# Routing tables in PSUM, a divisor out of the matmul, and another order of scatters and weight splits, in a fused attention and mixture-of-experts kernel

## The chip, the cores and the metric

The kernel runs on one core of a Trainium2 chip. The metric is the device time of one execution in microseconds.

## The reference

Three parts follow one another. Attention has 4 batches, 8 heads, 576 tokens, 64 columns; k and v are averaged over groups of 8 tokens first, so there are 72 keys.

```python
scores = scale * np.matmul(q, k_p.transpose(0, 1, 3, 2))
scores = scores - np.max(scores, axis=-1, keepdims=True)
attn = np.exp(scores)
attn = attn / (np.sum(attn, axis=-1, keepdims=True) + 1e-09)
return np.matmul(attn, v_p).astype(np.float32)
```

Its output is a matrix x of 2304 tokens by 512. Each token then goes to two of 8 experts: logits are `x @ w_gate`, plus noise times `log1p(exp(x @ w_noise))`; the two largest win; their weights are a softmax over the two. An expert is `relu(x @ w1) @ w2` with 1024 hidden columns. The last part is dense, with 2048 hidden columns: `h = x @ w_in`, then `max(0.01 * h, h) @ w_out`.

## The kernel before, in words

Every matmul of the experts and of the dense part is made of three (`halves3`, L663 to L667): each fp32 operand is split into a high half that TensorE takes exactly and the rest. Weights are split by GpSimd, in 16 chunks of 128x512 for each of ten stages (eight experts, two dense halves), out of a ring of four raw chunks (`w_raw`) that SP loads. A split is a TENSOR_SCALAR and a TENSOR_TENSOR (`split_chunk` L451, `split_next` L493). Activations are split by ScalarE and VectorE.

**Attention** works on 18 tiles of 128 tokens in a pipeline of steps: at step t TensorE scores tile t (`score`), turns the probabilities of t-1 and attends for t-2 (`attend`); VectorE centres t (`centre`: maximum and subtraction), pools k and v by reductions (`pool_k`, `pool_v`, L1026 and L1034) and normalises t-2 (`normalise`, L1050); ScalarE takes the exponentials and copies. The gate matrices are folded into the pooled v (`map_v`), so that `attend` gives each head's output, its share of the gate logits, and a column that sums the probabilities, since the last columns of `v_pool` hold 1.0. `normalise` adds 1e-9 to that sum and multiplies by 8 (L1053), takes the reciprocal (L1056), and makes the rows of x (L1058) and the products for the gates (L1062).

**Routing** goes by turns of 6, 5, 4 and 3 tiles, in four steps on VectorE: `gate` adds the products over the heads; `pick_first` (L1084) and `pick_second` (L1104) find the two experts, in 17 small operations, each waiting for the one before it (`link`); after TensorE's `rank` counts the picks, `place` (L1124) gives each row its slot in the DRAM buffer `x_sorted`, where every expert has a region. GpSimd then scatters the rows with one indirect DMA for each tile and pick (`send_rows`, L462), 36 in all, two at a time, with a weight split between pairs. The steps at which each part of a turn runs are in the tables at the end (L1384 to L1395); in a step of VectorE's loop (L1157) the order is centring, placing, pooling, normalising, gating, picking. The last turn's picks and placing come after the loop. Stage 1's split weights lie over `x_rows` in SBUF, so a chunk may be split only when the tile under it is sent.

**The order of the first blocks** is set by semaphores. SP waits until the scatters of turns 0 and 1 have landed, tells `early_landed`, loads two weight chunks, does the same for turn 2 (`mid_landed`), loads two more, and waits for turn 3 (L407 to L419). ScalarE loads the rows of block 0 and 1 after `early_landed`, block 2 after `mid_landed`, and all others after the last scatter (L933 to L958). VectorE works out the lists of blocks (L1215 to L1245) behind `split_rows(0)`, in one queue ahead of `split_h(0)`, on one partition of 45 x 8 elements for the larger ones. `need_rows` finds out whether a block's rows have been placed.

**Experts** follow as 43 blocks of 128 rows: `up`, the turning of the next rows (L672), `down` of the block before, `turn_h`. Their results go to `y_blocks`, and are gathered back and mixed during the dense part, which runs in five groups of tokens.

## Time and profile before

| | us |
|---|---|
| median of 3 runs | 1077.89 (1076.13 to 1080.1) |
| the profiled execution | 1074.86 |
| its span | 1072.8 |
| TensorE busy | 1035.0 |
| GpSimd busy | 380.1 |
| VectorE busy | 378.0 |
| ScalarE busy | 272.8 |

The span runs from the first to the last instruction of the profiled execution. Its own time is 2.1 us longer. Attention fills about the first 110 us, the first expert block begins near 120 us. A row of the timeline has the start, the duration, engine, line, operation, output and input, and in brackets how long the engine stood idle before it and for whom.

### The profile page before, as it was taken

To read this page: it belongs to the slowest core of one execution; us is meant where nothing else is said; L and a number is where in the kernel's file an instruction comes from. 1 tells how busy PE (TensorE), PEld (TensorE's weight loads), DVE (VectorE), ACT (ScalarE), POOL (GpSimd) and SP (SyncE) were. 2 spreads that over 40 slices of the span, in tenths; PEclk is the share of its full clock that TensorE was granted. 3 is DMA by queue.
4 is the path that set the end of the run, shared out by engine and by line. 5 is a ranking of instruction groups with operands and counts; after the bars stand their busy time and mean duration, and the time that the engine had idled before them with its cause. 6 is when DMAs were issued, how large, how long until landed. Compare 5 with 4: busy or idle time off the path is not lost.

```text
span 1072.8 us, 16321 instructions
## 1 busy us (share of the span) xinstructions
PE 1035.0 (96%) x5208; PEld 872.7 (81%) x5209; DVE 378.0 (35%) x679; ACT 272.8 (25%) x498; POOL 380.1 (35%) x414
## 2 busy tenths in 40 slices
PE   5988699999999999999999999999999999999998
PEld 5887578888888888888888887888888888888887
DVE  6987734222212212122121223643324333333222
ACT  4443112222222222222222221332222222222222
POOL 3338782552809164371908308801101100000000
PEclk9988689999999999999999999999999999999999
DMA  8944462341515233241514315311101101001001
GB/s 312 344 161 165 175 194 89 109 136 60 182 42 161 83 117 120 86 156 51 174 59 147 98 49 159 117 48 40 29 12 59 40 20 60 20 1 40 1 1 39
DMA packets 53926, 106.05 MB, mean 99 GB/s; under 512 B 7424, under 2 KB 7552, under 8 KB 53888
## 3 DMA queue, kind: packets, MB, share of 16 engines
q1 hardware_dynamic: 35456, 63.59, 18.5%
q10 hardware_dynamic: 12672, 23.07, 6.4%
q0 software_dynamic: 5760, 18.88, 5.2%
q8 instruction: 24, 0.39, 0.1%
q14 instruction: 14, 0.11, 0.0%
HBM read 77.47 MB, written 28.05 MB: 98 GB/s over the span
## 4 chain that ended last, share of the span: by engine, by line
PE 90%; DVE 7%; issue 2%; ACT 1%; DMA 0%; SPq 0%; DVEq 0%; ACTq 0%
PE ps L665 27%; PE ps L667 26%; PE ps L666 26%; PE ps L691 3%; PE ps L672 2%; PE ps L601 1%; PE ps L623 1%; DVE maxima L1040 1%; PE ps L779 1%; DVE v_sum L1034 1%; DVE k_sum L1026 1%; PE ps L611 1%; DVE x_rows L1058 0%; DMA k_raw<-in_kT_dram 0%; PE ps L588 0%
## 5 line engine op out<-in xcount | busy, mean ns | idle before, releaser
L502 POOL TENSOR_TENSOR w_split<-w_raw,w_split 128x512 fp32r<-128x512 f32 x144 | 186.7, 1297 | 12.0
L500 POOL TENSOR_SCALAR w_split<-w_raw 128x512 fp32r<-128x512 f32 x144 | 91.3, 634 | 214.7 <-PE ps L667 210.9
L665 PE MATMUL ps<-w_split,hT_hi 128*128 (+1 forms) x344 | 139.6, 406 | 2.7 <-DVE hT_lo L1198 2.7
L665 PE MATMUL ps<-w_split,xs_hi 128*128 (+1 forms) x344 | 138.4, 402 | 2.3 <-DVE xs_lo L1191 2.3
L667 PE MATMUL ps<-w_split,hT_lo 128*128 (+1 forms) x344 | 135.6, 394 | 0.0
L666 PE MATMUL ps<-w_split,hT_hi 128*128 (+1 forms) x344 | 135.0, 392 | 0.0
L666 PE MATMUL ps<-w_split,xs_hi 128*128 (+1 forms) x344 | 134.8, 392 | 0.0
L667 PE MATMUL ps<-w_split,xs_lo 128*128 (+1 forms) x344 | 134.7, 392 | 0.0
L548 POOL DMA_INDIRECT y_in<-y_blocks,y_rows x36 | 34.8, 966 | 254.3 <-DVE x L1326 201.2
L665 PE MATMUL ps<-x_hi,w_split 128*128 128x512 f32 (+1 forms) x320 | 119.4, 373 | 0.6 <-DVE x_lo L1359 0.6
L1371 DVE TENSOR_TENSOR g_sb<-h_small,ps 128x512 f32<-128x512 f32 (+1 forms) x80 | 50.7, 634 | 192.8 <-ACT h_small L1008 191.1
L666 PE MATMUL ps<-x_lo,w_split 128*128 128x512 f32 (+1 forms) x320 | 117.8, 368 | 0.0
L667 PE MATMUL ps<-x_hi,w_split 128*128 128x512 f32 (+1 forms) x320 | 117.8, 368 | 0.0
L665 PE MATMUL ps<-w_split,g_hi 128*128 128x512 f32 x288 | 112.4, 390 | 0.7 <-DVE g_lo L1374 0.7
L666 PE MATMUL ps<-w_split,g_hi 128*128 128x512 f32 x288 | 112.2, 390 | 0.0
L667 PE MATMUL ps<-w_split,g_lo 128*128 128x512 f32 x288 | 112.1, 389 | 0.0
L930 ACT ACTIVATE hT_hi<-ps 128x512 fp32r<-128x512 f32 x86 | 46.9, 596 | 256.0 <-PE ps L691 256.0
L1008 ACT ACTIVATE h_small<-ps 128x512 f32<-128x512 f32 (+1 forms) x80 | 44.4, 555 | 221.8 <-PE ps L667 221.7
L1191 DVE TENSOR_TENSOR xs_lo<-ps,xs_hi 128x512 fp32r<-128x512 f32 x44 | 30.4, 691 | 173.0 <-ACT xs_hi L918 173.0
L1207 DVE COPY y_sb<-ps 128x512 f32<-128x512 f32 x42 | 29.1, 692 | 171.9 <-PE ps L667 171.9
L924 ACT ACTIVATE h_sb<-ps 128x512 f32<-128x512 f32 x86 | 51.4, 598 | 150.2 <-PE ps L667 150.2
L665 PEld LDWEIGHTS ps<-w_split,hT_hi 128*128 128x128 f32 x344 | 65.2, 189 | 15.1 <-DVE hT_lo L1198 2.9
(165 smaller groups left out, 1512.5 us busy)
## 6 DMA issues: line engine op xcount, KB each, us to landing
w_raw<-in_wall_dram SPq DMA_DIRECT2D x160, 256.0 KB
xs<-x_sorted ACTq DMA_DIRECT2D x45, 256.0 KB
y_blocks<-y_sb ACTq DMA_DIRECT2D x43, 256.0 KB, 2.0
k_raw<-in_kT_dram SPq DMA_DIRECT2D x16, 288.0 KB, 5.2
q_sb<-in_qT_dram SPq DMA_DIRECT2D x18, 256.0 KB, 4.3
v_raw<-in_vT_dram SPq DMA_DIRECT2D x16, 288.0 KB, 4.7
out_dram<-h_sb SPq DMA_DIRECT2D x10, 256.0 KB, 2.0
x_sorted<-zero_rows SPq DMA_DIRECT2D x9, 256.0 KB, 4.2
```

Source lines behind the costliest of these rows:

```text
L500: pool.tensor_scalar(hi, w_raw[:, a, :], 1.0, 0.0, ALU.mult, ALU.add).then_inc(split_hi, 1)
L502: pool.tensor_tensor(lo, w_raw[:, a, :], hi.bitcast(F32), ALU.subtract).then_inc(split, 1)
L548: pool.indirect_dma_start(out=y_in[:, t % YRING, k, :], out_offset=None, in_=y_blocks[0:rows, :], in_offset=bass.IndirectOffsetOnAxis(ap=y ...
L665: pe.matmul(out_ap, lhs_hi, rhs_hi, start=first, stop=False)
L666: pe.matmul(out_ap, lhs_hi, rhs_lo, start=False, stop=False)
L667: return pe.matmul(out_ap, lhs_lo, rhs_hi, start=False, stop=last)
L691: mm = pe.transpose(ps[:, HT_BANK + n, k * P:(k + 1) * P], h_sb[:, (4 * n + k) * P:(4 * n + k + 1) * P], ident[:, :])
L924: act.activation(h_sb[:, n * BANK:(n + 1) * BANK], ps[:, H_BANK + n, :], ACT.Relu).then_inc(h_relued, 1)
L930: act.activation(hT_hi[:, 4 * n:4 * n + 4, :].rearrange("p a b -> p (a b)"), ps[:, HT_BANK + n, :], ACT.Copy).then_inc(hT_hi_made, 1)
L1008: act.activation(h_small[:, f % 2, 0:n], ps[:, H2_BANK + f % 2, 0:n], ACT.Copy, scale=0.01).then_inc(h2_small, 1)
L1191: dve.tensor_tensor(xs_lo[:, :, :].rearrange("p a b -> p (a b)"), ps[:, XT_BANK, :], xs_hi[:, :, :].rearrange("p a b -> p (a b)").bitcast( ...
L1371: dve.tensor_tensor(g_sb[:, f % 2, 0:n], h_small[:, f % 2, 0:n], ps[:, H2_BANK + f % 2, 0:n], ALU.max).then_inc(g_made, 1)
```

## The change

Five things are done.

1. The small tables of routing (`tmp`, `logit`, `noisy`, `rev`, the second maximum) and of the lists (`e8`, `at_end`, `row_if`, `region0`, `is_pick`) move from SBUF to free columns of PSUM bank 7 and bank 5, so that an operation mostly has one input in each memory. `rev` and `region0` are made in SBUF and copied once.
2. `pick_first` and `pick_second` move to right behind `centre` and `place` in a step, and one step later; `need_rows` is called at each `place`.
3. The sums column is 8.0 and a 73rd row of `v_pool`, met by ones in `probsT`, adds 8e-9 in the matmul, so `normalise` has only the reciprocal left. GpSimd fills these rows at the start. For the last tile the gates are made and summed before the rows of x.
4. GpSimd splits 12 chunks (8 before) ahead of the first scatter, then alternates three scatters with one split, and in turns 2 and 3 two with one. Splits of stage 1 begin within turn 1.
5. SP waits for each turn by itself (`x_sent_first`, `first_landed` are new), with three, four and two weight loads between; block 0 needs only turn 0.

The pooling of v has no line in the diff: VectorE does it before and after.

```diff
-EARLY_TURNS = 2
-EARLY_SENT = 2 * TURN_FROM[EARLY_TURNS]
-MID_SENT = 2 * TURNS[EARLY_TURNS]
+FIRST_SENT = 2 * TURNS[0]
+EARLY_SENT = 2 * TURNS[1]
+MID_SENT = 2 * TURNS[2]
+LATE_SENT = 2 * TURNS[3]
...
+        ranks, tmp, noisy, logit = (ps[:, G_BANK, n * one:(n + 1) * one].rearrange("p (t e) -> p t e", e=EXPERTS)
+                                    for n in range(4))
...
+        at_end = ps[0:1, AT_BANK + 1, 0:table].rearrange("p (b e) -> p b e", e=EXPERTS)
...
+            sp.wait_ge(x_sent_first, 16 * FIRST_SENT)
+            sp.sem_inc(first_landed, 1)
+            for n in range(CHUNKS + RING, CHUNKS + RING + 3):
+                load_w(n)
             sp.wait_ge(x_sent_early, 16 * EARLY_SENT)
             sp.sem_inc(early_landed, 1)
-            for n in range(CHUNKS + RING, CHUNKS + RING + 2):
+            for n in range(CHUNKS + RING + 3, CHUNKS + RING + 7):
                 load_w(n)
             sp.wait_ge(x_sent_mid, 16 * MID_SENT)
             sp.sem_inc(mid_landed, 1)
-            for n in range(CHUNKS + RING + 2, CHUNKS + RING + 4):
+            for n in range(CHUNKS + RING + 7, CHUNKS + RING + 9):
                 load_w(n)
...
+            rows = rows_of(0)
+            for n in range(SPLIT_FIRST, CHUNKS):
+                at = (n - SPLIT_FIRST) * 3
+                send_rows(0, rows[at:at + 3])
+                split_chunk(n)
+            rows = rows_of(1)
+            n = 0
+            for at in range(0, len(rows), 3):
+                send_rows(1, rows[at:at + 3])
+                if at + 3 < len(rows):
+                    pool.wait_ge(x_sent_first, 16 * FIRST_SENT)
+                    split_next(1, n, second_chunk(n), 2 * STAGE)
                     n += 1
...
+            rows = rows_of(3)
+            for at in range(0, len(rows), 2):
+                send_rows(3, rows[at:at + 2])
+                if at:
+                    pool.wait_ge(x_sent_mid, 16 * MID_SENT)
+                split_next(1, n, second_chunk(n), 2 * STAGE)
+                n += 1
...
-            act.wait_ge(first_known, 2)
-            load_early(0, early_landed)
+            act.wait_ge(first_known, 1)
+            load_early(0, first_landed)
...
-                dve.tensor_scalar(sums[:, 0, :].rearrange("p (a b) -> p a b", a=2), mixed[:, :, :, HCOLS], 1e-9, float(POOL),
-                                  ALU.add, ALU.mult).then_inc(summed, 1)
-                dve.wait_ge(summed, t * 2 + 1)
-                dve.reciprocal(sums[:, 1, :], sums[:, 0, :]).then_inc(summed, 1)
...
+                dve.reciprocal(shares[:, :].rearrange("p (a b) -> p a b", a=2), mixed[:, :, :, HCOLS]).then_inc(summed, 1)
...
+                if t < TILES - 1:
+                    make_rows()
+                    make_gates().then_inc(rows_made, 1)
+                else:
+                    make_gates().then_inc(last_gates_made, 1)
...
+                    make_rows().then_inc(rows_made, 1)
...
+            then(dve.tensor_scalar(nb_sb, end, 1.0, None, ALU.max))
             then(dve.tensor_scalar(nb, end, 1.0, None, ALU.max))
...
-SPLIT_FIRST = 8
+SPLIT_FIRST = 12
...
-GATE_AT = tuple(t + 2 for t in TURN_END)
-LOG_AT = FIRST_AT = tuple(t + 3 for t in TURN_END[:-1])
-SECOND_AT = tuple(t + 4 for t in TURN_END[:-1])
-GAP_AT = tuple(t + 5 for t in TURN_END[:-2])
+GATE_AT = tuple(t + 2 for t in TURN_END[:-1])
+LOG_AT = tuple(t + 3 for t in TURN_END[:-1])
+FIRST_AT = tuple(t + 4 for t in TURN_END[:-1])
+SECOND_AT = tuple(t + 5 for t in TURN_END[:-1])
+GAP_AT = tuple(t + 6 for t in TURN_END[:-2])
```

## Rows read from the trace of the kernel before

**Rows 1.** The page: busy time of TensorE; shares of the chain that ended last, by engine.
```profile
PE 1035.0 (96%) x5208; PEld 872.7 (81%) x5209; DVE 378.0 (35%) x679; ACT 272.8 (25%) x498; POOL 380.1 (35%) x414
...
PE 90%; DVE 7%; issue 2%; ACT 1%; DMA 0%; SPq 0%; DVEq 0%; ACTq 0%
```

**Rows 2.** Windows of 20 us: busy us of each engine (x instructions), clock, DMA share, GB/s.
```profile
40.00:60.00 20.00, 16.94 (x127) 15.88 (x126) 19.04 (x47) 8.16 (x18) 7.55 (x8) 0.86 0.84 308
```

**Rows 3.** Groups by line, VectorE, whole span: busy us, mean ns of one, idle before.
```profile
L1053 DVE TENSOR_SCALAR sums<-ps 128x8 f32<-128x8 f32 x18 | 2.8, 158 | 6.0 <-PE ps L623 3.8 <-issue 2.2
...
L1099 DVE TENSOR_TENSOR tmp<-logit,top 128x48 f32<-128x48 f32 (+3 forms) x4 | 2.0, 505 | 0.1
L1100 DVE TENSOR_TENSOR tmp<-tmp,rev 128x48 f32<-128x48 f32 (+3 forms) x4 | 1.9, 473 | 0.1
...
L1096 DVE TENSOR_TENSOR logit<-gates_sb,tmp 128x48 f32<-128x48 f32 (+3 forms) x4 | 1.2, 303 | 0.1
...
L1095 DVE TENSOR_TENSOR tmp<-z_abs,noise_sb 128x48 f32<-128x48 f32 (+3 forms) x4 | 1.1, 285 | 0.1
...
L1129 DVE TENSOR_TENSOR tmp<-ps,row_of 128x48 f32<-128x48 f32 (+3 forms) x4 | 0.8, 190 | 2.0 <-issue 2.0
```

**Rows 4.** Timeline, VectorE: start us, us, line, operation.
```profile
81.30 1.08 DVE L1099 TENSOR_TENSOR tmp<-logit,top 128x40 f32<-128x40 f32 x1
```

**Rows 5.** Timeline, GpSimd: splits of weight chunks and row scatters.
```profile
16.70 0.62 POOL L458 TENSOR_SCALAR w_split<-w_raw 128x512 fp32r<-128x512 f32 x1 [10.57 <-DMA w_raw<-in_wall_dram]
...
71.46 0.63 POOL L458 TENSOR_SCALAR w_split<-w_raw 128x512 fp32r<-128x512 f32 x1
...
75.91 0.63 POOL L458 TENSOR_SCALAR w_split<-w_raw 128x512 fp32r<-128x512 f32 x1
...
81.06 1.27 POOL L460 TENSOR_TENSOR w_split<-w_raw,w_split 128x512 fp32r<-128x512 f32 x1
...
143.11 0.96 POOL L468 DMA_INDIRECT x_sorted<-x_rows,slots_i  x1 [0.30 <-issue]
145.96 0.62 POOL L500 TENSOR_SCALAR w_split<-w_raw 128x512 fp32r<-128x512 f32 x1 [1.89 <-issue]
```

**Rows 6.** Timeline, VectorE: the lists of blocks.
```profile
122.06 0.90 DVE L1215 TENSOR_TENSOR e<-row_of,region 128x8 f32<-128x8 f32 x1
...
126.72 1.50 DVE L1232 TENSOR_TENSOR probsT<-probsT 1x360 f32<-1x360 f32 x1
128.26 0.52 DVE L1233 SCALAR_TENSOR_TENSOR probsT<-bnum,e 1x360 f32<-1x360 f32 x1
...
131.55 1.23 DVE L1243 CAST block_expert<-rows_f 1x45 int32<-1x45 f32 x1
```

**Rows 7.** Timeline, TensorE: a score, and the first two expert blocks.
```profile
86.51 2.08 PE L601 MATMUL ps<-k_pool,q_sb 128*128 128x144 f32 x8
...
122.20 0.80 PE L665 MATMUL ps<-w_split,xs_hi 128*128 128x512 f32 x1 [1.48 <-DVE xs_lo L1191]
...
133.75 0.80 PE L665 MATMUL ps<-w_split,hT_hi 128*128 128x512 f32 x1 [2.69 <-DVE hT_lo L1198]
...
139.03 0.88 PE L672 MATMUL ps<-ident,xs 128*128 128x128 f32 x4
...
155.86 0.60 PE L672 MATMUL ps<-ident,xs 128*128 128x128 f32 x4
```

**Rows 8.** Timeline, ScalarE and its DMA queue around the first two blocks.
```profile
130.25 0.59 ACT L930 ACTIVATE hT_hi<-ps 128x512 fp32r<-128x512 f32 x1
...
134.35 0.35 ACTq L942 DMA_DIRECT2D xs<-x_sorted  x1
```

**Rows 9.** Timeline, SP's DMA queue: weight loads after the last load of q.
```profile
75.64 20.38 SPq L333 DMA_DIRECT2D w_raw<-in_wall_dram  x6
```

**Rows 10.** The page: DMA issues, count, KB each, median us to landing.
```profile
y_blocks<-y_sb ACTq DMA_DIRECT2D x43, 256.0 KB, 2.0
...
q_sb<-in_qT_dram SPq DMA_DIRECT2D x18, 256.0 KB, 4.3
```

More of the change, by code:

```diff
@@ L138, in build @@
         before = sb("before", [P, P])
-        rev = sb("rev", [P, TURN_MAX, EXPERTS])
+        rev_sb = sb("rev_sb", [P, TURN_MAX, EXPERTS])
         row_of = sb("row_of", [P, EXPERTS])
-        region0 = sb("region0", [P, EXPERTS])
+        region0_sb = sb("region0_sb", [P, EXPERTS])
         jpad = sb("jpad", [P, EXPERTS, TILES])
@@ L144, in build @@
         bnum = sb("bnum", [1, LISTED, EXPERTS])
-        z_abs, z_exp, z_log, logit, tmp, picked = (
-            sb(n, [P, TURN_MAX, EXPERTS]) for n in ("z_abs", "z_exp", "z_log", "logit", "tmp", "picked"))
+        z_abs, z_exp, z_log, second, picked = (
+            sb(n, [P, TURN_MAX, EXPERTS]) for n in ("z_abs", "z_exp", "z_log", "second", "picked"))
         picks = sb("picks", [P, 2, TURN_MAX, EXPERTS])
@@ L485, in _ @@
                                pattern=[[1, EXPERTS], [-1, EXPERTS]], channel_multiplier=0).then_inc(consts_made, 1)
-            count(rev[:, :, :], [[0, TURN_MAX], [-1, EXPERTS]], EXPERTS, 0)
+            count(rev_sb[:, :, :], [[0, TURN_MAX], [-1, EXPERTS]], EXPERTS, 0)
             count(row_of[:, :], [[REGION, EXPERTS]], 0, 0)
-            count(region0[:, :], [[REGION, EXPERTS]], 0, 0)
+            count(region0_sb[:, :], [[REGION, EXPERTS]], 0, 0)
             count(jpad[:, :, :], [[0, EXPERTS], [P, TILES]], 0, 0)
@@ L529, in _ @@
             pool.wait_ge(x_sent_mid, 16 * MID_SENT)
-            pool.wait_ge(x_sent_late, 16 * (2 * TILES - EARLY_SENT - MID_SENT))
-            for c in range(n - CHUNKS, CHUNKS):
+            pool.wait_ge(x_sent_late, 16 * LATE_SENT)
+            for c in range(n, CHUNKS):
                 split_next(1, c, second_chunk(c), 2 * STAGE)
@@ L868, in copy_v @@
                     act.wait_ge(attended, LAST_TILE[b - 2] + 1)
[L869 removed]
+                if 2 * b + half == 0:
+                    act.wait_ge(eps_made, 1)
+                act.activation(v_pool[0:KEYS, b % 2, 4 * half:4 * half + 4, 0:HCOLS],
                                v_turned.rearrange("p a (h c) -> p (a h) c", c=HCOLS),
@@ new lines, in normalise, with by_column, make_rows @@
+                dve.wait_ge(summed, t + 1)
+                r = max(q for q in range(len(TURNS)) if TURN_FROM[q] <= t)
+                def by_column(n):
+                    return shares[:, :].rearrange("p (a b) -> p a b", a=2).unsqueeze(3).to_broadcast([P, 2, HEADS // 2, n])
+                def make_rows():
+                    return dve.tensor_tensor(x_rows[:, t, :].rearrange("p (a b d) -> p a b d", a=2, d=HD),
+                                             mixed[:, :, :, 0:HD], by_column(HD), ALU.mult)
@@ L1161, in _ @@
                     place(PLACE_AT.index(step))
-                    if PLACE_AT.index(step) == EARLY_TURNS - 1:
-                        need_rows(0)
-                        need_rows(1)
+                    need_rows(PLACE_AT.index(step))
+                if step in FIRST_AT:
+                    if step == FIRST_AT[0]:
+                        dve.wait_ge(consts_in, 16)
+                        dve.wait_ge(consts_made, MADE)
+                        link(dve.tensor_copy(rev, rev_sb[:, :, :]))
+                        link(dve.tensor_copy(region0, region0_sb[:, :]))
+                    pick_first(FIRST_AT.index(step))
+                if step in SECOND_AT:
+                    pick_second(SECOND_AT.index(step))
                 for u in K_AT.get(step, ()):
@@ L1253, in by_expert @@
                     return x.unsqueeze(3).to_broadcast([P, TILES, 2, EXPERTS])
-                then(dve.scalar_tensor_tensor(out=first_moved, in0=nb, scalar=float(P), in1=region0[:, :],
+                then(dve.scalar_tensor_tensor(out=moved_sb, in0=nb_sb, scalar=float(P), in1=region0,
                                               op0=ALU.mult, op1=ALU.add))
-                then(dve.tensor_scalar(first_moved, first_moved, -float(P), None, ALU.add))
-                then(dve.tensor_tensor(moved, first_moved, last_row, ALU.subtract))
+                then(dve.tensor_scalar(first_moved, moved_sb, -float(P), None, ALU.add))
+                then(dve.scalar_tensor_tensor(out=moved, in0=moved_sb, scalar=-float(P), in1=last_row,
+                                              op0=ALU.add, op1=ALU.subtract))
                 then(dve.tensor_tensor(to_y, by_expert(slots_f[:, :, :]), of_picks(first_moved), ALU.is_ge))
```

149 lines of the change are left out of this document (79 added, 70 removed).

## The prediction

> **What bounds the kernel now.** I read the engine table and the chain of waits first [rows 1]: TensorE is busy 96% of the span and 90% of the chain runs through it. From the third expert block on nothing but those matmuls counts, and the change touches none of them. So it can pay only by letting that unbroken stretch begin sooner. The window of 40 to 60 us [rows 2] shows who is ahead of it: VectorE is busy 19.04 of 20 us there, in a stage where TensorE waits for its reductions. After attention come a few serial microseconds, with TensorE idle or at half clock.
>
> The second reading is why VectorE is slow. In the groups by line [rows 3] a small routing operation costs 190 ns when one input is in PSUM (L1129), but 505, 473, 303 and 285 ns on average at L1099, L1100, L1096 and L1095, which read two tensors in SBUF. One instance [rows 4] starts at 81.30 and takes 1.08; GpSimd's subtraction of 1.27 from 81.06 [rows 5] ends at 82.33, and VectorE's ends 0.05 later. So these operations are held until GpSimd is done.
>
> The Trainium skill, "GPSIMD Engine Reference", table of the engine's properties, says that its SBUF interfaces are shared, with contention for VectorE instructions of two SBUF inputs or in a 2-port mode. By that the casts that the change leaves in SBUF stay exposed, three of them at the end of the lists; were each held for a whole subtraction, the term of the lists below would fall from 2.1 to under 1 us and the sum by as much. The trace agrees in kind, at L1243, a cast of 45 elements that took 1.23 us [rows 6]; but that is one such case, and it was there before as well, so the term stays as the rows give it.
>
> **Part by part.** *Tables in PSUM, picks.* The four lines at four turns lose 4 x ((505 + 473 + 303 + 285) - 4 x 190) ns = 3.2 us. No row shows VectorE writing PSUM; nearest is L1129, which reads it at 190 ns [rows 3]. From above, a write could cost as much again, 0.2 each; from below it is nothing, or a little gain that I know no reason for and can't exclude. I take nothing, as in that nearest row. Two new copies (`rev`, `region0`) cost 2 x 0.19 = 0.4.
>
> *Divisor from the product.* L1053 goes: 18 x 158 ns = 2.8 us [rows 3]. It had 6.0 us of idle time before it in all, so some of it lies under a TensorE wait: I count 12 of 18, 1.9 us (bounds 0 and 2.8). The matmul of `attend` gets a 73rd row of the contraction, which adds no column: nothing. The three new GpSimd fills at the start lie in the 10.57 us that it waits before its first split [rows 5]; nothing, and a few us of delay would be covered too.
>
> *Picks behind the next centring.* The picks of turns 0 and 1 move one step later, ahead of the pooling. This hands TensorE its scores sooner but leaves the same work in the two steps together; what is late next is `rank`, queued ahead of `score` on TensorE. I take nothing. The exposed cast of `place(1)`, which now falls while GpSimd is still scattering turn 0, may wait from nothing to 1.0 (the 1.23 of L1243 [rows 6] less a small operation's 0.19): I take 0.5.
>
> *Clock.* The score before `centre(15)` ran at half clock, 2.08 us for 8 matmuls, after TensorE had stood waiting for a pooled v [rows 7]; that comes sooner now. Between 0 and 1.0 us back, I take 0.8.
>
> *Last turn.* The gates go first, `make_rows` behind them. `place(2)` after them still waits for `rank(2)`, which TensorE runs behind `attend(17)`: nothing. Pooling of v is by VectorE before and after: the diff has no line for it.
>
> Sum to the first `up`: 3.2 + 1.9 - 0.4 - 0.5 + 0.8 = 5.0 us before 122.20 [rows 7].
>
> *Lists.* They run from 122.06 while block 0's `up` runs. Excess of [rows 6]: 0.90 against 0.19 at L1215; 1.50 against 0.52 at L1232; two more of that width I put at 0.3 each by the same reasoning. 0.7 + 1.0 + 0.6, less 0.2 for the doubled `nb`: 2.1 us. TensorE stood 2.69 us before 133.75 for the hT_lo that is queued behind the lists [rows 7]. The first half of ScalarE's hT_hi was ready at 130.25 + 0.59 = 130.84 [rows 8], and hT_lo's half takes about 0.7 before TensorE starts at 133.75, so the lists hold it back by 133.75 - 0.7 - 130.84 = 2.2. The saving fits under that. I take 2.1, bounds 1 and 2.7.
>
> *After it.* From 133.75 to 139.03 twelve matmuls took 0.44 us each [rows 7], half clock (1.2 GHz), where the full one (2.4 GHz) would give 0.22. With a shorter idle stretch before them 2.5 us may come back. But `turn_rows(1)` at 139.03 needs block 1's rows, whose load was issued at 134.35, 1.3 us after the lists and behind `copy_h(0)` [rows 8]; with its landing this caps the return. I take 0.5.
>
> Together TensorE would reach the rows of block 3, at 155.86 before [rows 7], 5.0 + 2.1 + 0.5 = 7.6 us sooner.
>
> *Scatters and splits in turn.* This is the part that can cap it. Those rows wait for the very last scatter. Before, it ended at 143.11 + 0.96 = 144.07, and GpSimd saw it landed 1.89 later [rows 5]. After: four more splits stand ahead of turn 0. The splits past them wait for chunk 12, which SP issues behind `q(17)`, at 75.64 before [rows 9], hence about 73.3 now (2.3 of the gain is made by then). A load of this size took 4.3 us to land (q_sb) or 2.0 (y_blocks) [rows 10]; that stage is q's, so 77.6. Behind it come 33 scatters at 0.96 + 0.30 = 1.26 and 13 splits at 4.45 - 2 x 1.27 = 1.91 (two scatters and a split take 71.46 to 75.91) [rows 5]: 41.6 + 24.8 = 66.4, end 144.0. So the last scatter does not get earlier at all. Landed 145.9; SP, the registers and ScalarE's issue add 0.9, the rows themselves 2.0 (by y_blocks, of the same stage): 148.8. TensorE would want them at 155.86 - 7.6 = 148.3. It waits some 0.5 us, and the gain is capped near 7.0. With q's 4.3 for the rows the cap is 4.8. I take 6.5.
>
> SP's new wait for turn 0 stands ahead of chunk 20, when turn 0 has long landed; `mid_landed` now comes behind chunks 23 to 26, that is after seven of the second stage's splits: 77.6 + 27 x 1.26 + 11 x 1.91 = 132.6. Even with 0.9 and 4.3 behind that block 2's rows are there at 137.8, and TensorE wants them between `down(0)` and `up(2)`, near 140. ScalarE's wait for the last scatter has `store_rows(0)`, `copy_h(1)` and `relu(2)` behind it, each needed only after those rows. Three more loads and the splits of the second expert finish sooner than before, and are not waited for.
>
> So 1074.86 (the profiled execution, 1072.8 of span and about 2 around it) becomes 1068.4. The median of the runs shown is 1077.89, 3.0 above that execution; the same 6.5 us makes 1071.4.
>
> **The rivals.** *Nothing caps it.* The rows land quickly and the clock stays up: for it speaks that y_blocks, of the same size and stage, landed in 2.0 and that my landing of chunk 12 is the slow one. Then the 7.6 stand, with the clock's 2.5 in place of 0.5, up to 9.6 us: 1069 with the middle of that.
>
> *The late scatter costs more.* VectorE's and GpSimd's leftovers collide, the rows arrive at 151 and TensorE, after standing 2 us or more, starts again at half clock, as it did at 133.75. The cap gives 5, twelve slow matmuls take 2.5 back: 1075.4.
>
> *The freed VectorE time is not the bound.* The idle time that ended at TensorE in attention [rows 3] grows, and only the lists pay: gain 2 to 3, 1075.
>
> *Writing PSUM is dear.* This is the one that ends slower. 32 operations of the picks and some 12 of the lists now write PSUM, nearly all on the serial path. At 0.15 us more each, 44 x 0.15 = 6.6, the gain is gone: that is the point from which it decides. At 0.3 each, 13.2 us, the end is 6.7 later, 1084.6. Against it: reading PSUM is as cheap as SBUF (190 ns), and no step on this engine scales with the place of its operand in any row that I see.
>
> **How the numbers follow.** A measurement here can tell about 0.5%, 5.4 us, from no change. Forecast (cap near 6.5, spread 5 to 7.3) 0.40; nothing caps it 0.20; late scatter costs more 0.20; not the bound 0.14; dear PSUM 0.06. Faster by over 0.5%: three quarters of the first, all of the second, a fifth of the third: 0.54. Slower by over 0.5%: most of the last, 0.05. Within: 0.41. The range leaves out the last and the far end of the fourth: 1066.5 to 1077.5.
>
> **What would show it.** L1099's and L1100's successors near 0.2 us at every turn; L1243's not. No operation in the place of L1053. First `up` near 117.2, `down(0)` near 126.6 with under 1 us of idle time before it. Last scatter ending near 144, as before. TensorE waiting under 2 us at the transposes of block 3, near 149, and unbroken from there. A small operation writing PSUM at 0.3 us or more, or the last scatter past 150, would make the forecast wrong; so would `up(0)` after 120.

## The result, and the profile after

| | before | after |
|---|---|---|
| median, us | 1075.99 (1072.25 to 1082.33, 20 runs) | 1079.56 (1075.0 to 1084.89, 20 runs) |
| the profiled execution | 1074.86 | 1075.12 |
| its span | 1072.8 | 1073.2 |

The ratio is 1.0032, 95% interval 1.0019 to 1.0046: 0.3% slower, under the 0.5% that the prediction took for the least that a measurement can tell. A later comparison of the same two kernels gave 1.0007 (0.999 to 1.0025), with a median of 1076.25. The forecast was 6.5 us faster, 1071.4, with a range up to 1077.5; 1079.56 lies 2.1 above the range. What stands firm over both comparisons is that the gain is missing; whether the kernel is slower than before is not. The executions that were profiled lie near each other, so they show where the expected gain went, but not the whole of the 3.6 us between the medians, whose cause is open. One execution of all, 1085.02 us in sends_again below, counts as a slow one and is left out of its ratio.

The page of the changed kernel, span and engines. VectorE has lost 12.8 us of work against [rows 1], and the time has not moved.

```profile
span 1073.2 us, 16314 instructions
...
PE 1036.3 (97%) x5208; PEld 873.4 (81%) x5209; DVE 365.2 (34%) x664; ACT 272.3 (25%) x498; POOL 383.1 (36%) x417
```

The groups by line of VectorE in the changed kernel: busy us, mean ns, idle before. L1152, L1153, L1156 and L1157 are what was L1095, L1096, L1099 and L1100 in [rows 3]. All four write PSUM and take 200 to 204 ns, where L1129 took 190.

```profile
L1150 DVE SCALAR_TENSOR_TENSOR ps<-gates_sb,z_log 128x48 f32<-128x48 f32 (+3 forms) x4 | 1.7, 431 | 0.0
...
L1157 DVE TENSOR_TENSOR ps<-ps,rev_sb 128x48 f32<-128x48 f32 (+3 forms) x4 | 0.8, 204 | 0.1
L1152 DVE TENSOR_TENSOR ps<-ps,noise_sb 128x48 f32<-128x48 f32 (+3 forms) x4 | 0.8, 204 | 0.1
L1156 DVE TENSOR_TENSOR ps<-ps,top 128x48 f32<-128x48 f32 (+3 forms) x4 | 0.8, 203 | 0.1
...
L1153 DVE TENSOR_TENSOR ps<-gates_sb,ps 128x48 f32<-128x48 f32 (+3 forms) x4 | 0.8, 200 | 0.1
```

VectorE's timeline in the lists, the same places as [rows 6]: 0.16 for 0.90, 0.52 for 1.50, and in this execution the cast, still in SBUF, 0.18 for 1.23.

```profile
122.35 0.16 DVE L1274 TENSOR_TENSOR ps<-row_of,ps 128x8 f32<-128x8 f32 x1
...
125.89 0.52 DVE L1292 TENSOR_TENSOR probsT<-probsT,ps 1x360 f32<-1x360 f32 x1
...
129.62 0.18 DVE L1303 CAST block_expert<-rows_f 1x45 int32<-1x45 f32 x1
```

So the parts that make operations shorter do what they say. Next is VectorE at step 10 of the changed kernel: the picks of turn 0 run from 57.69, behind the centring, and the poolings that TensorE needs come behind them, as they did before. The second fence has the pooled v of the kernel before: it was ready at 62.74 there, and is at 61.69 now, so it comes no later.

```profile
57.69 0.19 DVE L1167 SCALAR_TENSOR_TENSOR second<-picks,ps 128x48 f32<-128x48 f32 x1
...
59.63 1.40 DVE L1070 TENSOR_REDUCE k_sum<-k_raw 128x72 f32<-128x576 f32 x2
60.95 0.74 DVE L1078 TENSOR_REDUCE v_sum<-v_raw 128x72 f32<-128x576 f32 x1
...
68.03 0.76 DVE L1084 TENSOR_REDUCE maxima<-ps 128x8 f32<-128x576 f32 x1 [5.21 <-PE ps L639]
```

```profile
62.00 0.74 DVE L1034 TENSOR_REDUCE v_sum<-v_raw 128x72 f32<-128x576 f32 x1
```

TensorE over the same stretch, and then at the first expert blocks. It stands 3.20 us for the pooled v; then `map_v`, `rank` and `score(11)` run one after the other at half clock (L673's ten matmuls take 2.27 us, where the kernel before took 1.25). Meanwhile VectorE stands 5.21 us. `map_v` begins 1.06 us sooner than before (62.80, second fence) and `centre(11)` 1.88 later (68.03, before 66.15): from the one to the other 6.29 us for 3.35. Before, TensorE's stand came a step earlier: 2.47 us until 55.64, and `score(10)` behind it ran at half clock (2.26 us). The new order moves the stand more than it makes one.

```profile
56.56 1.98 PE L661 MATMUL ps<-v_pool,probsT 73*128 73x82 f32 x16 [0.90 <-DVE gate_prod L1109]
61.74 1.34 PE L626 MATMUL ps<-v_to,v_sum 128*72 128x160 f32 x4 [3.20 <-DVE v_sum L1078]
...
63.18 2.27 PE L673 MATMUL ps<-picked,ones 128*128 128x40 f32 x10
...
65.72 2.27 PE L639 MATMUL ps<-k_pool,q_sb 128*128 128x144 f32 x8
...
122.49 0.80 PE L704 MATMUL ps<-w_split,xs_hi 128*128 128x512 f32 x1 [1.48 <-DVE xs_lo L1249]
...
132.67 0.50 PE L704 MATMUL ps<-w_split,hT_hi 128*128 128x512 f32 x1 [0.56 <-DVE hT_lo L1256]
...
156.23 0.60 PE L711 MATMUL ps<-ident,xs 128*128 128x128 f32 x4
```

```profile
62.80 0.76 PE L588 MATMUL ps<-v_to,v_sum 128*72 128x160 f32 x4
```

The window of 60 to 66 us, first of the changed kernel (busy us of TensorE, its weight loads, VectorE, ScalarE, GpSimd, then the granted clock), then of the kernel before: 0.50, the lower level of 1.2 GHz, against 0.91.

```profile
60.00:66.00 6.00, 4.26 (x19) 4.19 (x20) 2.79 (x6) 1.69 (x6) 1.60 (x3) 0.50 0.29 93
```

```profile
60.00:66.00 6.00, 5.88 (x47) 5.66 (x46) 4.07 (x8) 2.96 (x7) 0.00 (x0) 0.91 0.33 109
```

Third, the loads and the scatters. SP's queue issues the last two loads of q, each after the score that frees its buffer, and chunk 12 behind them at 77.60.

```profile
72.66 4.90 SPq L338 DMA_DIRECT2D q_sb<-in_qT_dram  x2
77.60 69.74 SPq L349 DMA_DIRECT2D w_raw<-in_wall_dram  x17
```

GpSimd in the changed kernel: it stands 4.45 us for chunk 11, 4.01 us for chunk 12, and issues the last scatter 5.35 us later than in [rows 5].

```profile
71.48 0.62 POOL L488 TENSOR_SCALAR w_split<-w_raw 128x512 fp32r<-128x512 f32 x1 [4.45 <-DMA w_raw<-in_wall_dram]
...
81.40 0.62 POOL L488 TENSOR_SCALAR w_split<-w_raw 128x512 fp32r<-128x512 f32 x1 [4.01 <-DMA w_raw<-in_wall_dram]
...
148.46 0.96 POOL L498 DMA_INDIRECT x_sorted<-x_rows,slots_i  x1 [0.30 <-issue]
```

**A ruler for all runs.** From block 4's transposes on all kernels are alike: the span ends 904.7 us (904.65 to 904.77) after their start, in each of the 16 profiled executions. So a profile can be judged by when that point is reached (168.12 before, 168.49 after), and everything is decided ahead of it.

### The profile page after: what moved, and what is told of

Read it like the earlier page. It is cut to its first block, busy times and chain, and to the rows that moved or that the text cites. A ratio compares the mean times of both kernels' runs of the same rounds, so it can differ in the third digit from the quotient of the medians.

```text
span 1073.2 us, 16314 instructions
## 1 busy us (share of the span) xinstructions
PE 1036.3 (97%) x5208; PEld 873.4 (81%) x5209; DVE 365.2 (34%) x664; ACT 272.3 (25%) x498; POOL 383.1 (36%) x417
## 4 chain that ended last, share of the span: by engine, by line
PE 90%; DVE 5%; issue 2%; DMA 1%; ACT 1%; SPq 0%; ACTq 0%; DVEq 0%
PE ps L704 27%; PE ps L706 26%; PE ps L705 26%; PE ps L730 3%; PE ps L711 2%; PE ps L639 2%; PE ps L661 2%; PE ps L649 1%; DVE maxima L1084 1%; DVE v_sum L1078 1%; PE ps L818 1%; DMA k_raw<-in_kT_dram 1%; DVE k_sum L1070 0%; DVE x_rows L1105 0%; DMA xs<-x_sorted 0%
## 5 line engine op out<-in xcount | busy, mean ns | idle before, releaser
L704 PEld LDWEIGHTS ps<-w_split,xs_hi 128*128 128x128 f32 x344 | 65.4, 190 | 15.2 <-DVE xs_lo L1249 1.9
```

The source lines that it names most:

```text
L704: pe.matmul(out_ap, lhs_hi, rhs_hi, start=first, stop=False)
```

## The experiments

Two theories, and they can both hold. **P**: the picks behind the next centring move TensorE's stand in step 10 to right ahead of `rank` and `score(11)`, which then run at half clock, and this costs about what the shorter operations give. **S**: the new order of scatters, splits and chunk loads delays the last scatter, so that block 3's rows are late. The rivals: the tables, the divisor or the last turn cost something themselves; or neither part matters, and the gain was never there, since VectorE was not the bound.

In the table, all times are us on the profiled execution's clock. The wait in brackets is TensorE's, before block 3's transposes. after_look was executed once and has no ratio.

| kernel | ratio (95%) | first `up` | `down(0)` | last scatter ends | block 3 | block 4 |
|---|---|---|---|---|---|---|
| before | 1 | 122.20 | 133.75 | 144.07 | 155.86 | 168.12 |
| after | 1.0032 (1.0019, 1.0046) | 122.49 | 132.67 | 149.42 | 156.23 | 168.49 |
| after_again | 1.0007 (0.999, 1.0025) | 120.52 | 130.56 | 148.97 | 154.96 [3.94] | 169.50 |
| after_look | | 123.41 | 133.31 | 150.29 | 157.79 [3.70] | 172.25 |
| picks_back | 1.0001 (0.9982, 1.002) | 118.35 | 127.97 | 146.73 | 154.77 [6.09] | 169.73 |
| sends_back | 1.0018 (0.9984, 1.0053) | 125.49 | 135.28 | 145.72 | 156.66 | 168.89 |
| sends_again | 0.9988 (0.9962, 1.0015) | 123.24 | 133.11 | 143.75 | 154.44 | 166.67 |
| both_back | 0.9956 (0.9932, 0.998) | 122.30 | 132.70 | 143.37 | 155.82 | 168.09 |
| both_again | 0.9936 (0.9909, 0.9962) | 118.56 | 129.02 | 141.63 | 149.40 | 161.63 |
| filler | 1.0011 (0.9995, 1.0026) | 121.09 | 131.24 | 148.92 | 154.76 [3.23] | 169.93 |
| warm_sends | 0.9951 (0.9921, 0.998) | 118.59 | 127.92 | 141.27 | 148.26 | 160.53 |
| tables_sbuf | 0.9985 (0.9964, 1.0005) | 120.72 | 132.28 | 141.51 | 152.32 | 164.55 |
| w12_pb | 0.9968 (0.9953, 0.9983) | 127.53 | 137.20 | 150.22 | 157.40 | 169.67 |
| early_pb | 0.9999 (0.998, 1.0019) | 118.33 | 136.70 | 131.54 | 157.46 | 169.69 |
| early_late_picks | 1.0045 (1.002, 1.007) | 122.74 | 139.27 | 132.81 | 161.43 | 173.70 |
| early_pb_warm | 1.0017 (0.9996, 1.0039) | 129.07 | 139.02 | 135.86 | 159.61 | 171.84 |

### One part undone, and both

**picks_back**: the picks again behind pooling, normalising and gating, and one step earlier.

```diff
+                pool k, pool v, normalise, gate
                 if step in FIRST_AT: pick_first(...)
                 if step in SECOND_AT: pick_second(...)
-                pool k, pool v, normalise, gate
-FIRST_AT = tuple(t + 4 for t in TURN_END[:-1])
+FIRST_AT = tuple(t + 3 for t in TURN_END[:-1])
```

> The changed kernel with both picks back behind pooling, normalising and gating, and one step earlier; all else stays. Theory A (the move of the picks costs the attention stage: TensorE stood 3.2 us before the last pooled v of step 10 and then ran rank(0) and score(11) at half clock, with VectorE waiting 5.2 us for them): VectorE's idle time before centre(11) falls from 5.2 to about 2 us, centre(11) begins near 64 instead of 68.0, and the first up near 119. The end gains only if the last scatter also comes earlier (its first follows slots_ready or the 12th split): theory A alone says 3 to 5 us below the changed kernel, near 1075. Rival B (the last scatter, at 149.4 instead of 144.1, decides): the end stays within 1.5 us of the changed kernel, 1079, and TensorE gains a wait at the rows of block 3.

**sends_back**: only the order of scatters, splits, SP's waits and chunk loads as before (`SPLIT_FIRST` 8, pairs of scatters); block 0 still needs only turn 0. **both_back**: both edits.

> The changed kernel with the order of scatters, splits and SP's waits and loads of before (8 splits first, pairs, no split of the next stage before the last turn's slots); picks stay late. Theory A: no gain in attention, first up stays near 122 and the time stays at 1078 to 1080, although the last scatter ends near 146. Rival B: the last scatter comes 4 us sooner and the end with it, 1075 or less.

> Both of these put back; what is left of the change is the tables in PSUM, the reciprocal alone and the last turn's order. If both theories hold in part, only this one shows the 5 us that the first stage should have gained: first up near 117 to 118, list wait gone, about 1070. If the tables and the divisor are worth nothing (the freed VectorE time lies under waits), 1076, like before.

Both undone gave 0.9956: the rest of the change is worth 0.44% in that comparison, 4.7 us. Its profiled execution, at 1074.49 us one of the two slowest of eight, doesn't show the gain: the first `up` was expected at 117 to 118 and came at 122.30. Either edit alone gave nothing that can be told from no change. In picks_back `centre(11)` began at 65.82 (near 64 expected) and the first `up` at 118.35 (near 119 expected), with the wait at block 3 that the rival had named. TensorE's timeline says why the one without the other is worthless: the first `up` comes 3.85 us sooner than before, `down(0)` 5.8 sooner, and then it stands 6.09 us for the rows of block 3.

```profile
154.77 1.12 PE L711 MATMUL ps<-ident,xs 128*128 128x128 f32 x4 [6.09 <-DMA xs<-x_sorted]
```

GpSimd in that kernel: 5.05 us for chunk 12, and the last scatter. The next split that needs the scatters landed comes only at 151.00, ScalarE's load of block 3's rows at 151.61.

```profile
80.09 0.62 POOL L488 TENSOR_SCALAR w_split<-w_raw 128x512 fp32r<-128x512 f32 x1 [5.05 <-DMA w_raw<-in_wall_dram]
...
145.77 0.96 POOL L498 DMA_INDIRECT x_sorted<-x_rows,slots_i  x1 [0.30 <-issue]
...
151.00 0.62 POOL L529 TENSOR_SCALAR w_split<-w_raw 128x512 fp32r<-128x512 f32 x1 [2.24 <-DMA x_sorted<-x_rows,slots_i]
```

both_back and sends_back were run once more.

> The same kernel as both_back (the changed kernel with the picks and the order of scatters, splits and chunk loads as before), once more with more rounds: theory 0.9956 again, 0.993 to 0.998, the last scatter near 143.4; if the first result was luck it comes out at 0.998 or above.

> The same kernel as sends_back, once more, because four of its twelve times lay 12 us above the rest. Theory: near 1.000 without such runs, centre(11) near 68 to 69 us. If the far group belongs to the order of scatters, it comes again here and in the kernel with the idle matmuls; if it belongs to the chip, the kernel before shows it in this call too.

both_again came out at 0.9936, 1067.16 us against 1075.46: this program beat the kernel before twice. It doesn't do so in every execution: nine of its twelve times are 1063.35 to 1069.06, the other three 1072.99 to 1076.13, at mean granted clocks of 0.986 to 0.990 and 0.979 to 0.982. TensorE's timeline of both_again, whose profiled execution is one of the nine: block 3's transposes no longer wait, and the point of the ruler is reached 6.5 us before 168.12. Its profiled span is 6.4 us shorter.

```profile
118.56 0.80 PE L695 MATMUL ps<-w_split,xs_hi 128*128 128x512 f32 x1 [1.48 <-issue]
...
149.40 0.60 PE L702 MATMUL ps<-ident,xs 128*128 128x128 f32 x4
161.63 0.60 PE L702 MATMUL ps<-ident,xs 128*128 128x128 f32 x4
```

sends_again lies 0.52% above both_again in the same comparison: that is the price of the picks once the scatters are not in the way. The four times near 1085 us of sends_back (the rest near 1073) lift its ratio to 1.0018; such times came again twice in sends_again (1083.08 and 1085.02), with a mean clock of 0.97, and not among the 35 of before in that comparison, whose longest was 1082.54. What makes them was not found.

**Where the picks cost.** The stand in step 10 isn't the whole of it. Centrings mark the time on VectorE; each stretch below holds the same picks in either order. Times are us from one centring to the other, then to the first `up`.

| kernel | picks | 8 to 11 | 11 to 13 | 13 to 16 | 16 to first `up` |
|---|---|---|---|---|---|
| both_again | back | 20.46 | 9.77 | 14.78 | 25.79 |
| sends_again | late | 21.30 | 9.78 | 17.63 | 27.20 |
| early_pb | back | 20.03 | 9.85 | 14.90 | 25.66 |
| early_late_picks | late | 21.10 | 9.76 | 17.62 | 26.59 |
| picks_back | back | 17.91 | 10.02 | 14.77 | 27.74 |
| after | late | 20.33 | 9.77 | 18.05 | 26.64 |

In the first two pairs more than half of the price, 2.7 to 2.9 us, arises in steps 13 to 16, and about 1 up to step 11. For in both_again TensorE ran `rank` and `score(11)` at half clock too, behind a stand of 0.94 us, with the picks back:

```profile
62.49 0.78 PE L617 MATMUL ps<-v_to,v_sum 128*72 128x160 f32 x4 [0.94 <-DVE v_sum L1069]
...
63.37 2.27 PE L664 MATMUL ps<-picked,ones 128*128 128x40 f32 x10
```

The later stretch goes with the clock. VectorE's centrings 15 and 16 in sends_again, then in both_again: 7.57 us from one to the other, and 3.64. The granted clock of sends_again was 0.76 from 84 to 90 us and 0.78 from 90 to 96; the third fence has both_again's 84 to 96, at 1.00.

```profile
88.47 0.76 DVE L1075 TENSOR_REDUCE maxima<-ps 128x8 f32<-128x576 f32 x1 [1.29 <-PE ps L630]
...
96.04 0.76 DVE L1075 TENSOR_REDUCE maxima<-ps 128x8 f32<-128x576 f32 x1 [2.23 <-PE ps L630]
```

```profile
89.13 0.74 DVE L1075 TENSOR_REDUCE maxima<-ps 128x8 f32<-128x576 f32 x1
...
92.77 0.76 DVE L1075 TENSOR_REDUCE maxima<-ps 128x8 f32<-128x576 f32 x1 [0.49 <-PE ps L630]
```

```profile
84.00:96.00 12.00, 10.74 (x105) 10.30 (x104) 10.57 (x29) 4.63 (x7) 10.39 (x12) 1.00 0.51 177
```

The clock isn't bound to the order of the picks alone. It was 1.00 there in after_again and sends_back, with the picks late (13 to 16: 15.82 and 15.95 us), and 0.73 from 84 to 90 in both_back, with them back (16.33). So the price of the picks is measured; that it is paid in these two stretches is what the profiles show; why the clock fell in one execution and not in another is open.

### TensorE kept at work

**filler** adds 26 idle matmuls of 128 columns to the changed kernel, ahead of `map_v` in step 10; **warm_sends** adds 12 of them to sends_back.

```diff
+                if step == RANK_AT[0]:
+                    pe.wait_ge(centred, step + 1)
+                    for _ in range(26):
+                        pe.matmul(ps[:, S_BANK, HEADS // 2 * KEYS:HEADS // 2 * KEYS + P], ident[:, :],
+                                  ident[:, :], start=True, stop=True)
                 if step in VMAP_AT:
```

> The changed kernel with 26 idle matmuls of 128 columns on TensorE where it stands still in step 10, written to free columns of a scores bank; they compute nothing that is used. If the half clock of rank(0) and score(11) comes from that standing still, both run at full clock: rank 3.1 to 1.6 us, score 2.3 to 1.2, centre(11) near 65.3 instead of 68.0, the end up to 2.7 us sooner, 1077. If the clock does not come from it, nothing moves but for the matmuls themselves.

> The changed kernel with the old order of scatters, splits and chunk loads, and 12 idle matmuls of 128 columns (0.21 us each, 2.5 us) on TensorE ahead of map_v in step 10; the earlier filler had 26 of them, 6.0 us, and so held map_v to 64.82 us where pooled v was ready at 61.7. Theory (the picks' price is the stand of TensorE and the half clock in which rank and score(11) then run in the open): PEclk 1.00 from 60 to 68 us, score(11) starts near 63.3 and centre(11) near 65.3 where the changed kernel has 68.03, first up near 120; about 2.5 us less than the old-order kernel without them, ratio to before near 0.999. Rival (the picks cost by VectorE's time alone, whatever the clock): centre(11) stays at 68 and the ratio at 1.0018.

filler's timeline of TensorE: the stand is gone, and L673 takes 1.25 us again. From `map_v` to `centre(11)` it took 3.29 us where the changed kernel took 6.29: that is what the half clock costs there. But the matmuls were too many. They held `map_v` from 61.7 to 64.82, and what the clock gave back was spent on them; `centre(11)` began at 68.11, not near 65.3, and the ratio of 1.0011 can't be told from that of the changed kernel.

```profile
58.97 6.01 PE L696 MATMUL ps<-ident 128*128 128x128 f32 x52
64.82 0.71 PE L626 MATMUL ps<-v_to,v_sum 128*72 128x160 f32 x4
...
65.52 1.25 PE L673 MATMUL ps<-picked,ones 128*128 128x40 f32 x10
```

warm_sends gave 0.9951 (0.9921 to 0.998) against sends_again's 0.9988 (0.9962 to 1.0015), and its idle matmuls are the only difference. The intervals overlap: a gain is likely but not shown. The expected place was missed: its 12 matmuls ran at half clock themselves and took 4.90 us, so `centre(11)` began at 68.0 once more. What differs in the profiles comes later. The windows of 84 to 90 us, of warm_sends and then of sends_again:

```profile
84.00:90.00 6.00, 4.56 (x51) 4.36 (x52) 4.96 (x16) 2.12 (x4) 5.07 (x6) 1.00 0.46 146
```

```profile
84.00:90.00 6.00, 4.45 (x25) 3.76 (x24) 4.43 (x13) 0.87 (x2) 5.28 (x6) 0.76 0.40 141
```

The clock stayed at 1.00 from 66 to 102 us in the first; in the second it fell again, though TensorE's stand for a pooled v near 86 us was the same in both (1.53 and 1.55), and the first `up` came 4.65 us later. That isn't shown to be the work of the idle matmuls: sends_back, the same program as sends_again, ran at 1.00 from 84 to 96 us without them, as after_again did from 84 to 102.

### The tables alone

**tables_sbuf**: both_back with the tables in SBUF, all else kept.

```diff
-        ranks, tmp, noisy, logit = (ps[:, G_BANK, ...] for n in range(4))
+        ranks = ps[:, G_BANK, 0:one]...
+        tmp, noisy, logit = (small[:, n * one:(n + 1) * one]... for n in range(3))
+        small = sb("small", [P, 3 * TURN_MAX * EXPERTS + 64 + TURN_MAX])
```

The other tables (`rev`, `region0`, `e8`, `next_top`, `is_pick`, `row_if`, `at_end`) go back to SBUF with them, and the two copies go.

> Like both_back (picks and sends back), with the routing and list tables in SBUF as before: what is left is the reciprocal alone, the 73rd row and the last turn's order. If the tables in PSUM are what both_back gained 0.44% by, this is at 1075 to 1076, L1156 and L1157 are held by GpSimd again for up to 1.3 us, and TensorE stands over 2 us before down(0). If the tables are worth nothing, it is like both_back, 1071 to 1072.

0.9985 (0.9964 to 1.0005) against 0.9956 and 0.9936 with them in PSUM; the first pair of intervals overlaps, the second just does not, and both_back and both_again were measured in other comparisons. So that the tables bring most of the gain is likely; what the reciprocal and the last turn's order bring, 0.15% here, can't be told from nothing. TensorE stood 1.75 us before `down(0)`, where over 2 was expected and 0.56 is seen with the tables in PSUM. In its groups by line of VectorE the held operations are back, at other lines than before: where one falls depends on when GpSimd subtracts.

```profile
L1153 DVE TENSOR_TENSOR picks<-rev_sb,code 128x48 f32<-128x48 f32 (+3 forms) x4 | 2.4, 592 | 0.1
L1161 DVE SCALAR_TENSOR_TENSOR second<-picks,small 128x48 f32<-128x48 f32 (+3 forms) x4 | 2.0, 506 | 0.0
...
L1282 DVE TENSOR_TENSOR probsT<-bnum,small 1x360 f32<-1x360 f32 x1 | 1.5, 1492 | 0.0
```

### The load of chunk 12

**w12_pb**: picks_back, new order kept, but chunk 12's load ahead of the last two of q.

```diff
             load_w(11)
+            load_w(12)
             load_q(16)
             load_q(17)
-            for n in range(12, CHUNKS + RING):
+            for n in range(13, CHUNKS + RING):
```

> picks_back (new order of scatters and splits kept) with chunk 12's load issued ahead of the loads of q 16 and 17 on SyncE's queue. Theory (the new order's price is the one wait of GpSimd for chunk 12, 5.05 us at 80.09, because its load stands behind q loads that wait for scores): the wait goes, the last scatter ends near 141.7 us where picks_back has 146.73, block 3's rows are there by 150 and TensorE stands under 2 us before their transposes; time near both_back's, ratio 0.995. Rival (the alternation with splits or the third load wait is the price): the last scatter stays past 144.5 and the ratio near 1.000.

0.9968 (0.9953 to 0.9983) against picks_back's 1.0001: moving one load gives back 0.33%. The whole new order had cost 0.45% by both_back (0.9956) and 0.65% by both_again (0.9936), and w12_pb lies 0.32% above both_again, with which it was compared directly. So the load is about half or more of the price of the order, and the rest of it is not accounted for. The trace doesn't show it cleanly. The profiled execution was the slowest of its twelve (1076.3 us; the median is 1071.54), its scores ran at half clock from 64 to 82 us, and so the q loads held chunk 13 as they had held chunk 12. SP's queue and then GpSimd in w12_pb:

```profile
67.27 0.91 SPq L349 DMA_DIRECT2D w_raw<-in_wall_dram  x2
73.94 8.51 SPq L338 DMA_DIRECT2D q_sb<-in_qT_dram  x2
```

```profile
86.49 0.62 POOL L489 TENSOR_SCALAR w_split<-w_raw 128x512 fp32r<-128x512 f32 x1 [4.54 <-DMA w_raw<-in_wall_dram]
```

The expected end of the last scatter, 141.7, was missed there (150.22). So the price of the load is supported by the times; its path is seen in picks_back and after alone. The rival, that the alternation or the third load wait is the price, can't be ruled out for the rest.

### All scatters first

**early_pb**: picks_back with all 36 scatters in pairs, and no split of stage 1 before the last of them. **early_late_picks**: the same order with the change's picks. **early_pb_warm**: early_pb with 20 idle matmuls ahead of the last `rank`.

```diff
+            for turn in range(len(TURNS)):
+                rows = rows_of(turn)
+                for at in range(0, len(rows), 2):
+                    send_rows(turn, rows[at:at + 2])
+                    if n < CHUNKS:
+                        split_chunk(n)
+                        n += 1
+            pool.wait_ge(x_sent_first, 16 * FIRST_SENT)
+            pool.wait_ge(x_sent_early, 16 * EARLY_SENT)
```

> Picks back as in picks_back; and the scatters of turns 1 to 3 without a split between them once the 16 chunks of the first expert are split: all 36 scatters, then all 16 splits of the second expert. SP gives its four signals before it loads chunk 20. Theory (the last scatter is what took the gain in picks_back, where TensorE stood 6.1 us at block 3's rows and ran the next 10 matmuls at half clock): last scatter ends near 132 instead of 146.7, no wait at block 3's rows, its transposes near 151 to 152 instead of 154.8, the end 1070 to 1072, 4 to 6 us below before. Rival (the wait at block 3 is not from the last scatter but from something else on ScalarE's queue): still a wait of some us there and 1075. The second expert's splits end near 163, 20 us before they are wanted: no wait for them.

> The same order of scatters with the picks left as the change has them, behind the next centring. With the scatters out of the way the picks' own price shows: if it is the clock and the wait in steps 10 and 15, first up stays near 122 and the end is 3 to 4 us above early_pb, 1074 to 1076. If the picks cost nothing, both are alike.

> early_pb with 20 matmuls of 128 columns that compute nothing that is used, on TensorE between rank(2) and rank(3), where it stood 4.7 to 6.1 us. If the half clock of up(0)'s first 9 matmuls comes from that standing, they run at full clock, rank(3) and the transposes of block 0 too: 2 to 3 us below early_pb, near 1068. If not, like early_pb.

The last scatter ended at 131.54 in early_pb, 15 us sooner, TensorE no longer stood before block 3's transposes, and yet the ratio was 0.9999: these began at 157.46, where 151 to 152 was expected. TensorE has a new stand there, between the first `up` and `turn_h(0)`:

```profile
125.34 0.39 PE L685 MATMUL ps<-w_split,xs_lo 128*128 128x512 f32 x1
132.54 1.12 PE L709 MATMUL ps<-ident,h_sb 128*128 128x128 f32 x4 [6.82 <-issue]
```

The ReLU before it, on ScalarE, started at 131.89, though its matmuls were done by 125.7, and stood for nothing that the profile shows:

```profile
131.89 0.60 ACT L946 ACTIVATE h_sb<-ps 128x512 f32<-128x512 f32 x1 [14.41 <-issue]
```

early_late_picks shows the same (5.73 us at 136.74) and measured 1.0045 (1.002 to 1.007), 0.46% above early_pb: the price of the picks a second time, under another order of scatters. early_pb_warm measured 1.0017 (0.9996 to 1.0039), with the first `up` at 129.07 and at half clock as before (near 1068 us expected, 1077.41 measured); its matmuls helped nothing. Why ScalarE stands is open. In both kernels the last 20 or so scatters follow one another without a break; early_pb_warm, with the same order but a pause of 3.90 us among them for the last `place`, has no such stand (0.25 us at the same place). That is a hint and no more; it was not taken further.

### The changed kernel again

> The changed kernel itself, once more. Its median of 1079.6 us lies 4.4 above the one execution that was profiled (1075.1, clock 0.981), so that profile may not show what the median pays. Theory (the picks leave TensorE standing in step 10 and the clock's answer differs from run to run): span stays the start of block 4's transposes plus 904.7 us; a slower execution has more half clock between 60 and 120 us and first up at 125 or later. Rival (the last scatter's lateness): first up stays near 122.5 and TensorE stands several us before block 3's transposes.

> The changed kernel, another profiled execution, for the same question: theory and rival as for after_again. If its time is near 1080, first up at 125 or later by the theory; near 122.5 with a stand before block 3's transposes by the rival.

Both profiled executions show both stands together; that the slower of them would reach the first `up` at 125 or later was not seen. after_look (1078.9 us) stood 3.62 us before `map_v`, reached the first `up` at 123.41, and stood 3.70 us before block 3's transposes. TensorE in after_again:

```profile
154.96 0.66 PE L711 MATMUL ps<-ident,xs 128*128 128x128 f32 x4 [3.94 <-DMA xs<-x_sorted]
```

At `down(0)` this execution is 3.2 us ahead of before, at block 3 0.9, at block 4 it is 1.4 behind: the matmuls after the stand follow each other at 0.43 us, at half clock, until 159.7. Block 3 to block 4 takes 14.54 us, before it took 12.26. In the first profile of the changed kernel TensorE was itself so late (156.23) that the rows did not show as a wait. Theories P and S both hold here in so far as this kernel pays the picks, and where it pays less for them, it runs into the late rows.

## Why the prediction was wrong, point by point

- **Tables in PSUM: right.** The four lines fell from 505, 473, 303 and 285 ns to 203, 204, 200 and 204, 3.0 us for 3.2 reckoned. The price of writing PSUM, taken as nothing, is nearly that: L1186, what was L1129, now writes PSUM and takes 192 to 206 ns where it took 183 to 196, 0.01 us more. With that the rival "writing PSUM is dear" is out.
- **The rest of the 5.0 us to the first `up`: seen once, and not the other time.** 122.20 became 118.56 in both_again, 3.6 us, in an execution whose `centre(0)` began 0.74 us later than that of before: 4.4. In both_back, the same program, it came at 122.30. The terms for divisor, clock and casts were not tried one by one; no run shows the divisor's 1.9 us or the clock's 0.8 by itself.
- **The first step that failed: "Picks behind the next centring ... I take nothing."** The prediction was right that VectorE has the same work in the two steps together: the pooled v comes no later than before. It was wrong that this makes the move free. It named `rank` as late next, and missed that TensorE, with its scores done sooner, stands for the pooled v of `map_v` right ahead of `rank` and `score(11)`, in one piece of 3.20 us (3.28 and 3.62 in the other two profiles), and runs both at half clock. Steps 13 to 16 cost more still. In the comparisons the picks' price is 0.52% (sends_again less both_again) and 0.46% (early_late_picks less early_pb), 5 to 5.6 us, or about the whole 5.0. How much of it is clock and how much is order stays open, since the half clock is also seen with the picks back.
- **Lists: a little less than reckoned.** TensorE's stand before `down(0)` fell from 2.69 to 0.56 us, after as in both_again. But more of `up(0)` ran at half clock: from `up` to `down(0)` 10.18 us after and 10.46 in both_again, where it was 11.55. So 1.1 to 1.4 for 2.1.
- **After it: from nothing to more than reckoned.** From `down(0)` to block 1's rows 3.8 us in both_again for 5.3 before, 1.5 and not 0.5, as the rows landed soon and the clock rose. In the first profile of the changed kernel TensorE stood 2.32 us for these rows and took 5.35, no gain. With both_again's 3.6, 1.1 and 1.5 and another 0.3 on the way to block 3 the sum is 6.5 us, where 7.6 uncapped was forecast.
- **The second step that failed: chunk 12 "hence about 73.3 now", the last scatter at 144.0.** On the clock of the span attention had gained nothing by then (`centre(12)` at 71.09 in picks_back, 71.28 before, though its `centre(0)` began 0.96 later) or had lost (73.06 after). The load was issued at 75.44 in picks_back and at 77.60 after, not 2.3 sooner than 75.64. From the chunk's split on the count of scatters and splits was right: 66.6 us in picks_back and 68.0 after for 66.4. So the scatter ended at 146.73 and 149.42.
- **The tail behind it** was put at 4.8 us from the last scatter's end to rows in SBUF; in picks_back it took 8.0, of which 4.3 went by until the scatters had landed (1.89 in [rows 5]) and 3.2 from ScalarE's issue to the transposes. The cap thus lay at 154.8 instead of 148.8. The rival "the late scatter costs more" described this mechanism, with its half clock behind it, but put the rows at 151.
- **"Freed VectorE time is not the bound" is out**: it put the gain at 2 to 3 us, and both_again's 0.9936 is 6.9, at least 4.1 by its interval, with 6.5 forecast. both_back's 0.9956 is 4.7.

The range ended at 1077.5, and the slower side had 0.05. Two costs that each take back the whole gain were not among the cases together.

The Trainium skill, "GPSIMD Engine Reference", properties table, names VectorE instructions of two SBUF inputs or in a 2-port mode as those that contend with GpSimd. The trace agrees in L1150, which kept two such inputs: at 82.42 us it took 1.02 us and ended at 83.44, just behind the subtraction of GpSimd (82.10 and 1.27 long); its mean is 431 ns where its neighbours, with one input in PSUM, have 200 to 204. The prediction's fear for the casts was borne out in part. In the first profile L1303 took 0.18, but in after_again its neighbour was held for 1.26 us, until 128.70, beside the subtraction of 127.37 to 128.66, and in picks_back for 1.23:

```profile
127.44 1.26 DVE L1302 CAST block_row<-rows_f 1x45 int32<-1x45 f32 x1
```

## What to carry to other kernels

Reordering two pieces of work on one engine can cost time even if their sum and what stands behind them stay the same: it moves the stands of the engine that waits. Follow that engine step by step, and price each stand together with the instructions right behind it, at the clock that rows show after such a stand. A load behind others on one queue inherits their waits: move it ahead of them before giving it a new early consumer. And when a change has several parts, measure the ones that shorten work apart from those that reorder it: here the first gave 0.4 to 0.6%, and with either of two reorderings alone no gain could be told from nothing.

## What the runs showed of the hardware that was not expected

- A stand can cost twice. After 3.94 us before block 3 the next nine matmuls ran mostly at the lower clock, and block 3 to block 4 took 2.28 us more than before. But its length alone doesn't tell: 0.94 us before `map_v` was followed by the lower clock in both_again and not in both_back, which is the same program; 1.55 us near 86 was followed by it in sends_again, 1.53 in warm_sends was not.
- Which VectorE operations are held beside GpSimd moves from build to build (L1099 and L1100 before, L1153 and L1161 in tables_sbuf), up to a mean of 592 ns where about 200 is usual. None of the routing TENSOR_TENSOR operations with one operand in PSUM was held in the traces: the successors of the four lines took 186 to 217 ns each in after, after_again, picks_back, both_back and both_again. Casts and operations of two SBUF inputs still were, `picked<-picks` in both_again for 1.15 us.
- One kernel's single profile can mislead by more than this change is worth: both_back and both_again are the same program, and reached block 4 at 168.09 and 161.63; their profiled executions took 1074.49 and 1068.05 us.
